# Chunk 0's k-times-v ahead of the gates' table, fewer filler matmuls in the sort, and 24 buffers for output rows

## What is computed

```python
# 1. linear attention: batch 4, 8 heads, 768 tokens, head width 64
for t in range(S):
    state = gamma * state + k[:, :, t] (outer) v[:, :, t]
    y[:, :, t] = scale * q[:, :, t] @ state
x = y as 3072 rows of 512
# 2. mixture of experts: each token goes to the expert with its largest gate logit
for e in range(8):
    mask = argmax(x @ w_gate) == e
    out[mask] = gate_w * eom * (relu(x[mask] @ w1[e]) @ w2[e])
# 3. soft mixture: 32 slots, softmax of (out @ phi) over the tokens makes the slots,
#    each slot goes through its expert, softmax over the slots mixes them back
return (c @ slot_out)          # 3072 rows of 512
```

## Time and profile before

| | us |
|---|---|
| median of 3 runs | 454.79 |
| the 3 runs | 452.96, 454.79, 454.80 |
| profiled execution, its own time | 454.17 |
| its span from first to last instruction | 452.2 |
| PE busy | 427.6 (95%) |
| attention loop ends near | 103 |
| first expert chunk's products begin near | 128.5 |
| first store of output rows is issued at | 427.9 |

### The profile page before, as it was taken

The page is one execution under the profiler, slowest core; times in us unless marked ns, Lnnn a source line. Parts: engine busy times, 40 slices in busy tenths (PEclk is TensorE's granted clock), DMA queues, the critical chain, the costliest instruction groups (busy, mean ns, idle before and its releaser), DMA issues.

```text
span 452.2 us, 10942 instructions
## 1 busy us (share of the span) xinstructions
PE 427.6 (95%) x4498; PEld 333.8 (74%) x4498; DVE 223.2 (49%) x448; ACT 154.7 (34%) x309; POOL 150.8 (33%) x144
## 2 busy tenths in 40 slices
PE   4969999999999999999999999999999999999980
PEld 4858888886576877977797798788779776644550
DVE  4656867677841444463554454454544623542141
ACT  2112221215332443444444443444444432211141
POOL 2442523220430437337335343363270170320000
PEclk9999999999699999999999999999999999999986
DMA  8999999998589579296495494692841976999998
GB/s 276 411 421 418 425 416 423 423 388 290 197 281 335 180 245 346 75 335 239 118 358 203 138 384 133 186 384 74 267 144 46 337 274 209 383 411 425 418 350 268
DMA packets 33394, 131.50 MB, mean 291 GB/s; under 512 B 5621, under 2 KB 12430, under 8 KB 26446
## 3 DMA queue, kind: packets, MB, share of 16 engines
q1 hardware_dynamic: 24558, 116.48, 68.3%
q0 software_dynamic: 5200, 7.95, 6.4%
q10 hardware_dynamic: 3600, 6.56, 3.8%
HBM read 117.66 MB, written 13.30 MB: 290 GB/s over the span
## 4 chain that ended last, share of the span: by engine, by line
PE 86%; DMA 7%; DVE 2%; SPq 1%; issue 1%; ACT 1%; DVEq 0%; ACTq 0%
PE bank L1446 12%; PE bank L1448 11%; PE bank L1447 11%; PE gbank L1329 5%; PE ybank L1379 4%; DMA qkv<-in_qkv 4%; PE bank L1352 4%; PE ybank L1557 3%; PE ybank L1538 3%; PE gbank L1513 3%; PE ybank L1513 3%; PE bank L1708 3%; PE ybank L1397 3%; PE ybank L1493 3%; DMA out<-orow 2%; PE ybank L1372 2%
## 5 line engine op out<-in xcount | busy, mean ns | idle before, releaser
L1446 PE MATMUL bank<-xT_hi,w_hi 128*128 128x432 f32 x256 | 97.5, 381 | 0.0
L1448 PE MATMUL bank<-xT_hi,w_lo 128*128 128x432 f32 x256 | 92.0, 360 | 0.0
L1447 PE MATMUL bank<-xT_lo,w_hi 128*128 128x432 f32 x256 | 91.9, 359 | 0.0
L656 POOL DMA_INDIRECT slot_logits<-lcur,logit_row_of_row x32 | 46.0, 1438 | 86.8 <-DVE lcur L1113 79.4
L763 ACT ACTIVATE hT<-bank 128x432 f32<-128x432 f32 x64 | 33.9, 529 | 104.6 <-PE bank L1448 90.5
L924 DVE TENSOR_TENSOR w_lo<-w_raw,w_hi 128x1024 fp32r<-128x1024 f32 x30 | 36.6, 1221 | 48.7 <-ACT w_hi L723 44.1
L1446 PEld LDWEIGHTS bank<-xT_hi,w_hi 128*128 128x128 f32 x256 | 48.1, 188 | 12.4 <-issue 10.1
L643 POOL DMA_INDIRECT xg<-x_rows,token_of_row x32 | 33.7, 1055 | 66.9 <-PE ybank L1463 38.8
L1447 PEld LDWEIGHTS bank<-xT_lo,w_hi 128*128 128x128 f32 x256 | 48.5, 190 | 1.8
L1448 PEld LDWEIGHTS bank<-xT_hi,w_lo 128*128 128x128 f32 x256 | 48.1, 188 | 2.3
L649 POOL DMA_INDIRECT gate_of_row<-gate_scales,token_of_row x32 | 33.0, 1030 | 29.1 <-DMA gate_scales<-gT 19.6
(11 more groups left out here) (216 smaller groups left out, 638.5 us busy)
## 6 DMA issues: line engine op xcount, KB each, us to landing
qkv<-in_qkv SPq DMA_DIRECT2D x21, 1024.0 KB, 13.8
w_raw<-in_w SPq DMA_DIRECT2D x32, 512.0 KB, 4.9
w<-in_w SPq DMA_DIRECT2D x8, 2048.0 KB
units<-in_v SPq DMA_DIRECT2D x12, 1024.0 KB, 14.2
units<-in_w2t SPq DMA_DIRECT2D x20, 512.0 KB, 10.4
units<-in_v SPq DMA_DIRECT2D x5, 2048.0 KB
x_rows<-xrow ACTq DMA_DIRECT2D x25, 256.0 KB, 7.2
units<-in_w2t SPq DMA_DIRECT2D x3, 2048.0 KB, 16.5
```

Source lines behind the costliest of these rows:

```text
L656: pool.indirect_dma_start(lt_d, bass.IndirectOffsetOnAxis(ap=at, axis=0), lcur[0:SUB, s, 0:SLOTS], None).then_inc(s_ltst, 16)
L1446: pe.matmul(out, wh, xh, start=first_, stop=False)
L1447: pe.matmul(out, wh, xl, start=False, stop=False)
L1448: return pe.matmul(out, wl, xh, start=False, stop=last_)
```

## The change

There are four edits. Line numbers of the changed file are lower by one up to the attention loop of PE, and higher by up to four behind it.

1. SP issues chunk 0's k,v rows ahead of `turn`.
2. In the first chunk of each batch (c = 0) PE now waits for `s_y` and does k times v ahead of `gates(i)`. In all other chunks nothing changes.
3. The fillers go from 6 to 3 ahead of `gates(T)` and from 4 to 2 ahead of the count matmuls.
4. There are 24 `orow` buffers, one for each output tile. 8 are in the place of `w2` as before, 8 in the place of `w1_raw`, 8 across the second half of `units[3]` and the first half of `units[4]` (numbered by `unit(n)`), all of which hold weights that have been used by then. The waits of the copies for earlier stores go.

```diff
-        e = unit(2)
-        orow = [put(f"orow{i}", [2, D // 2], at=e) for i in range(8)]
+        orow = []
+        for home in (unit(2), unit(1), [unit(3)[0] + 2 * UNIT]):
+            orow += [put(f"orow{len(orow) + i}", [2, D // 2], at=home) for i in range(8)]
...
         def keep_out(eng, b, r, done):
             eng.wait_ge(s_o[r], b + 1)
-            if b >= 2:
-                eng.wait_ge(s_out[b % 2 * 4 + r], 16 * (b // 2))
...
                     sp.dma_start(const[:, 0:N_FIRST], const_h[:, 0:N_FIRST]).then_inc(s_const, 16)
-                    sp.dma_start(turn[:, :, :], turn_h).then_inc(s_turn, 16)
                 sp.dma_start(qkv[i][:, 2:4, :], qkv_h[i][:, 2:4, :]).then_inc(s_kv[i], 16)
                 if i == 0:
+                    sp.dma_start(turn[:, :, :], turn_h).then_inc(s_turn, 16)
                     sp.dma_start(yscale[:, :, :], yscale_h).then_inc(s_ysc, 16)
...
-                    gates(i)
+                    if c > 0:
+                        gates(i)
+                    else:
+                        pe.wait_ge(s_y, i + 1)
                     if par < FIRST:
                         pe.wait_ge(s_kv[par], 16)
...
                         mm.then_inc(s_kvd, 1)
+                    if c == 0:
+                        gates(i)
                     for n in range(2):
                         pe.wait_ge(s_m, 2 * i + n + 1)
...
-            for _ in range(6):
+            for _ in range(3):
                 pe.matmul(bank[0][:, 0:P], turn[:, 0, 0:P], turn[:, 0, 0:P], start=True, stop=True)
             gates(T)
...
-            for _ in range(4):
+            for _ in range(2):
                 pe.matmul(bank[1][:, 0:P], ident, ident, start=True, stop=True)
```

More of the change, by code:

```diff
@@ L449, in keep_out @@
             eng.wait_ge(s_o[r], b + 1)
-            if b >= 2:
-                eng.wait_ge(s_out[b % 2 * 4 + r], 16 * (b // 2))
             src = bank[OUT_BANKS[OUT_SET[b]][r]][:, :].rearrange("p (t m) -> p t m", m=D // 2)
             if done is s_oea:
-                eng.activation(orow[b % 2 * 4 + r][:, :, :], src, ACT.Copy).then_inc(done, 1)
+                eng.activation(orow[4 * b + r][:, :, :], src, ACT.Copy).then_inc(done, 1)
             else:
-                eng.tensor_copy(orow[b % 2 * 4 + r][:, :, :], src).then_inc(done, 1)
+                eng.tensor_copy(orow[4 * b + r][:, :, :], src).then_inc(done, 1)
         block = ctx.enter_context(nc.Block())
@@ L602, in _ @@
                         sp.dma_start(out_h.rearrange("(u t r p) m -> u r p t m", p=P, r=4, t=2)[b % 3, r][:, :, b // 3 * D // 2:(b // 3 + 1) * D // 2],
-                                     orow[b % 2 * 4 + r][:, :, :]).then_inc(s_out[b % 2 * 4 + r], 16)
+                                     orow[4 * b + r][:, :, :]).then_inc(s_out[b % 2 * 4 + r], 16)
             for u in range(8):
```

## The result

| | before | changed |
|---|---|---|
| median (runs) | 454.86 (19) | 456.31 (19) |
| lowest and highest | 452.96, 456.5 | 453.58, 460.19 |
| profiled execution | 454.17 | 456.53 |
| its span | 452.2 | 454.7 |

The changed kernel takes 1.0038 of the time before, 95% interval 1.002 to 1.0055: some 1.7 us more, where I had forecast 0.2 less. The time lies in the range, and within 0.5%, but the direction was wrong. The head lost more than I allowed; the sort and the output stage won 0.85 and 0.6 on the mean of all traces, where I had 0.87 and 0.94.

A forecast was written before the change was run, and what follows sets the result against it. PE was taken to bound the middle, DMA engines the output stage. Head +1.9, sort -0.87 and output -0.94 gave +0.1 on 454.17: 454.3, or 454.9 from the median; the middle, 454.6, was forecast, range 452.6 to 456.4.

The forecast's parts named there:

- k,v rows 0.75 earlier: Head: with 288 KB moved behind them, chunk 0's k,v rows land 0.75 us earlier, POOL's k starting near 7.9; bounds 0 and 0.9.
- rival (d): Head: the order of two DMAs in flight does not bring the k,v rows forward; +0.75, 455.3; chance 0.09.
- The table lands "at or before 8.67": Head: the gates' table lands when the k,v rows did, ahead of the gates' start near 9.5, so costs nothing.
- The fill, +0.4 at full speed: Head: the gates now stand between k times v and AV, so AV starts at 10.7 instead of 10.27.
- The clock, +1.5 with an upper bound of 2.3: Head: PE's idle time delays the clock's rise; k times v, gates and half of AV run slow, +1.5; bounds 0 and 2.3.
- Rival (a): Head: the clock rises as early as before; sum -1.4, 453.2; chance 0.20.
- A late head pushes all of them: First pass through the loop: PE's instruction fetches follow its progress, so a late head delays all and reaches the end.
- Rival (b): Attention loop: instruction blocks do not depend on PE's progress, so idle time swallows the head's 1.9; 452.7; chance 0.13.
- Chunks 6, 12 and 18 at 0: Later batches' first chunks: k times v has the same wait for xT as the gates had; the new order costs 0.
- Edit 3, -0.87: Sort: with fewer fillers the count matmul starts at 107.38 instead of 108.25, -0.87; bounds -1.2 and 0.
- Rival (c): Sort: with five fillers fewer the clock falls earlier, ahead of 110; 2.5 more on PE, 457.1; chance 0.08.
- Edit 4, -0.94: Output stage: stores are bound by bandwidth, so only gaps in the DMA share are won, -0.94; bounds -1.3 and -0.3.

The follow-up runs named there:

- e1: Kernel before with only chunk 0's k,v rows issued ahead of the gates' table; ratio 1.0043.
- e14: Changed kernel with PE's old order restored (gates ahead of k times v in each batch's first chunk); ratio 1.0004 to the kernel before.
- e3: Kernel before with only the sort's fillers cut, from 6 to 3 and from 4 to 2; ratio 0.9996.
- e5: Kernel before with the fewer sort fillers and the 24 output-row buffers, without the two head edits; ratio 0.9942.
- e8: Kernel before with 24 output-row buffers, and the stores of DVE's tiles (12 of 24) issued by POOL instead of SP; ratio 0.9955.
- e4: Kernel before with only the 24 output-row buffers and no waits of the copies for earlier stores; ratio 0.998.
- e7: Kernel before with chunk 0's k,v rows loaded through ACT's queue instead of SP's; ratio 0.9969.
- e11: Changed kernel with the load order restored (table ahead of chunk 0's k,v rows); ratio 1.0026 to the kernel before.
- e2: Kernel before with only k times v put ahead of the gates in each batch's first chunk; ratio 1.0097.
- e6: e2 with the four gates matmuls run once more, unread, in PE's wait ahead of k times v; ratio 1.0089 to the kernel before.
- e12: e5 with chunk 0's k,v rows on ACT's queue and six filler matmuls ahead of chunk 0's scores; ratio 0.9957 to the kernel before.
- e13: e2 with six filler matmuls on PE ahead of chunk 0's scores; ratio 1.0037 to the kernel before.
- e10: Changed kernel, all four edits, with six filler matmuls on PE ahead of chunk 0's scores; ratio 1.003 to the kernel before.
- e16: e5 with six filler matmuls on PE ahead of chunk 0's scores; ratio 0.9931 to the kernel before, median 452.53.

## Why the prediction was wrong

The sum itself said +0.1 on the traced execution; the 0.2 less came from setting it between that and the median. What failed is the head: +1.9 stood there, and it cost 3.5 by the traces (2.8 and 0.67, below) and 4.4 by the ratios. Its lower bound of -0.4 doesn't follow from its terms either: +0.4 at full speed, with the 0.15 more that the landing could bring, is +0.3. The terms in turn:

**k,v rows 0.75 earlier: wrong, rival (d) was true.** I took the landing to follow the bytes ahead on the queue. In twelve traces with the table first, k_decayed starts at 8.44 to 9.57 (mean 8.8); in the four with the rows first at 8.96, 9.37, 8.05 and 8.95 (mean 8.8). So order on one queue brought the rows nothing on the mean; issued earlier and on a second queue, POOL could start at 6.35. The Trainium skill, "DMA: Bandwidth & Descriptors", "Queues, rings and completion order", says that completion isn't first in, first out within an issuing engine. No trace here shows that: these two loads landed in the order of their issue both ways.

**The table lands "at or before 8.67": wrong, and I had given it no price.** It landed at 9.8 in e1 and 9.4 in e14 and in the changed kernel, 7.3 to 7.7 us behind its issue, where it took 4.2 to 5.1 when issued ahead of the rows. In the changed kernel the new order hides that behind k times v, which ends at 11.1, so there it cost nothing; alone it costs 0.4%.

**The fill, +0.4 at full speed: right in kind.** The gates do stand between k times v and AV.

**The clock, +1.5 with an upper bound of 2.3: the step that failed most.** All of k times v, the gates and AV ran at the low level, 0.54 + 1.04 + 0.93 = 2.51, and chunk 1's scores with 0.37 more. I had taken half of AV and none of chunk 1. The head came out at +3.98 by chunk 1, where I had +1.9 with bounds to +2.7; the missing 2.1 are 1.04 of landing (k at 8.96, not 7.9) and 1.0 of low level. Part of the 3.98 belongs to the traced execution of before, whose level rose sooner than its siblings'. Against their median, 16.77, chunk 2 is 2.8 late, and in three of the four siblings (e3, e5, e8) k times v and AV ran at the low level too. So against the usual the loss is mostly the gates on the path, at 2.2 instead of the 1.18 of the full level, and not the slower k times v and AV.

Rival (a), "the clock rises as early as before", was false against the trace of before. That the hole made the rise late isn't shown, though. By the durations of the single matmuls the first rise came near 8.1, 11.7, 11.8, 13.4, 14.3 and 14.5 us where PE had no long hole (before, e4, e7, e3, e5, e8), near 13.3, 13.9, 15.4, 15.4 and 15.9 where it had one of 2.9 us or more (e11, e14, e1, e2, changed), and near 14.1 with the hole filled (e6). The means are 12.3 and 14.8, but single traces overlap, as AV of chunk 0 in e11 and in e5 shows:

```profile
12.80 1.26 PE L1383 MATMUL ybank<-masked_scores,qkv 128*64 128x128 f32 x16
```

```profile
10.55 1.92 PE L1378 MATMUL ybank<-masked_scores,qkv 128*64 128x128 f32 x16
```

**"A late head pushes all of them": right in the main.** From chunk 2's to chunk 6's scores it is 18.5 us within 0.3 in twelve of the eighteen traces, with chunk 2 anywhere from 15.1 to 19.5. Of the others e7 (20.31) and e12 (20.23) lost the clock within that stretch, before had 19.55, e5, e8 and e13 16.27, 17.91 and 17.89. In the pair of before and changed 1.04 of the 4.35 was swallowed, so a head earlier than usual isn't passed on whole. Rival (b) was false: the stops and the packets ahead of them move with PE. The Trainium skill, "Runtime: NRT & Kernel Launch", "Instruction fetch mechanics", calls the cost of a block's end mostly hidden; these traces have stops of 0.4 to 2.3 us for it, and there the measurement decides.

**Chunks 6, 12 and 18 at 0: wrong by 0.67.** I had looked only at what each part waits for, and there nothing changed. The matmuls themselves follow each other less tightly in the new order: 0.22 a chunk between starts, with no wait beside them. Why was not tried by itself.

**Edit 3, -0.87: right, with 0.86 at the count matmul.** At the first expert product 0.50 was left against the trace of before, which has the shortest stretch from the loop's end to that product of its kind. Over all traces that stretch is 25.5 to 26.0 with the old fillers and 24.7 to 25.3 with the new, so 0.85 on the mean. Rival (c) was false: the low level came 11.5 us behind the loop's end (11.0 before).

**Edit 4, -0.94: the right way, 0.6 on the mean.** In the pair of traces it was 0.17; from the first output tile to the end the mean is 26.9 over nine traces without it (26.0 to 28.6) and 26.3 over nine with it (25.7 to 26.8), 0.6 less. I had argued from one execution; more than half of the 0.6 is that the two bad cases, e3's 28.6 and e7's 27.8, have no like with 24 buffers. The gain alone, e4's 0.998, isn't clear of noise.

**The sum.** 2.8 + 0.67 - 0.85 - 0.6 = +2.0, and 1.7 was measured. By the ratios the head's two edits cost 4.4 us and the other two give 2.6 back, which is 1 us more on each side than the traces say. This difference stays open, and so does what e10's other executions did: the runs differ by 3 us, only one of each is traced, and the unedited middle alone varies by 2.

## What to carry to other kernels

Work that stands in an engine's wait isn't in the way, even where nobody needs it soon: before you move it behind the wait, ask what fills the hole, and on TensorE what the hole can do to the clock. Price it with every matmul up to the next rise at the low level, not with half of them. And moving a load ahead on its queue isn't the same as having it sooner; read the landings of several executions, issue it earlier, or give it a queue of its own, and look at what it delays there.

## What the runs showed of the hardware

- The time at which the level first rose differed by itself. With the same head, AV of chunk 0 took 1.05 in one trace and 1.57 to 1.92 in four, and chunk 2 started between 15.18 and 17.49. In 128 timed runs of the kernel before, the time goes with the recorded time at the low level in each run (a correlation of 0.54); that record begins behind the first rise, so this is the low level of the sort and the output stage and not of the head.
- A stop for instructions of about 2 us can be followed by the low level in the midst of a full loop (e7, 1.92 us and a fall at 32.34; e12, 2.26 us and a fall at 25.48), and chunk 2 to chunk 6 then took 20.3 and 20.2 us instead of 18.5. Stops of 2.00 (e16) and 1.82 (before) were not.
- Of two loads issued 0.46 us apart on one queue, with more behind them, the 288 KB one landed 4.2 to 5.1 us after its issue when first (twelve traces) and 6.4 to 7.7 when second (four). The 512 KB one took 6.0 to 7.1 when second and 6.1 to 7.4 when first. Issued at 0.74 on ACT's queue (e7, e12) it took 5.0.
